# One block for both programs, a moved load, masks before scans, a later first scoring and eight more unit products in a fused linear-attention and two-MLP kernel

## The reference

```python
for t in range(S):
    state = alpha[:, :, t, :, None] * state + np.einsum('bhd,bhe->bhde', k[:, :, t], v[:, :, t])
    y[:, :, t] = np.einsum('bhd,bhde->bhe', q[:, :, t], state)
x = attn_out.transpose(0, 2, 1, 3).reshape(B * S, H * D)
h = x @ w_in;  g = h * np.clip(h + 3.0, 0.0, 6.0) / 6.0;  x = g @ w_out      # first MLP
h = x @ w_in2; r = np.maximum(h, 0.0); g = r * r;         out = g @ w_out2   # second MLP
```

## Time and profile before

| what | us |
|---|---|
| median of three timed executions | 908.76 |
| lowest, highest | 907.75, 910.27 |
| the profiled execution | 911.25 |
| its span, first to last instruction | 909.5 |
| TensorE busy (PE) | 892.4 |
| VectorE, ScalarE, GpSimd busy | 331.5, 337.1, 312.1 |
| mean granted clock of TensorE | 0.994 of full speed |

### The profile page before, as it was taken

How to read it: one execution, slowest core, us unless ns; L and a number is a source line. 1 busy time by engine, 2 the same in 40 slices (tenths; PEclk the granted TensorE clock), 3 DMA queues, 4 the chain that set the end, 5 groups by cost and what they waited for, 6 DMA issues and landing times.

```text
span 909.5 us, 12748 instructions
## 1 busy us (share of the span) xinstructions
PE 892.4 (98%) x5036; PEld 738.7 (81%) x5036; DVE 331.5 (36%) x498; ACT 337.1 (37%) x600; POOL 312.1 (34%) x246
## 2 busy tenths in 40 slices
PE   7889999999999999999999999999999999999997
PEld 7778888888888888788888888888888888888886
DVE  7667454534634543554233331221221221211211
ACT  3544433424334333333344543332333422423332
POOL 2534244324334342533233333233332323333232
PEclk9899999999999999999999999999999999999999
DMA  9922204212222232030022300000000000000000
GB/s 300 308 55 72 70 21 106 58 54 54 56 56 52 54 108 56 18 90 5 5 100 74 105 0 1 35 1 1 35 1 1 35 1 0 36 1 1 35 1 36
DMA packets 22363, 47.70 MB, mean 52 GB/s; under 512 B 3616, under 2 KB 10016, under 8 KB 22304
## 3 DMA queue, kind: packets, MB, share of 16 engines
q1 hardware_dynamic: 22304, 46.89, 17.4%
HBM read 40.19 MB, written 4.72 MB: 49 GB/s over the span
## 4 chain that ended last, share of the span: by engine, by line
PE 95%; DMA 2%; DVE 1%; issue 1%; ACT 1%; SPq 0%; DVEq 0%; ACTq 0%
PE h_ps L745 43%; PE o_ps L758 43%; PE att_ps L700 2%; PE att_ps L665 2%; PE att_ps L703 2%; DMA x_mid<-att_in 2%; PE att_ps L676 1%; PE att_ps L719 1%; DVE w_in_lo L579 0%; PE att_ps L686 0%; PE o_ps L665 0%; PE o_ps L686 0%; ACT w_in_hi L443 0%; DVE h_act L561 0%; DVE masked_t L534 0%
## 5 line engine op out<-in xcount | busy, mean ns | idle before, releaser
L360 POOL TENSOR_TENSOR g_parts<-h_act,g_parts 128x512 fp32r<-128x512 f32 x192 | 252.6, 1316 | 572.1 <-ACT g_parts L426 572.1
L758 PE MATMUL o_ps<-g_parts,w_out_hi 128*128 128x512 f32 x1152 | 327.0, 389 | 0.0
L745 PE MATMUL h_ps<-x_parts,w_in_hi 128*128 128x512 f32 x1152 | 297.5, 393 | 0.2 <-ACT x_parts L401 0.2
L758 PEld LDWEIGHTS o_ps<-g_parts,w_out_hi 128*128 128x128 f32 x1152 | 216.2, 188 | 45.0
L745 PEld LDWEIGHTS h_ps<-x_parts,w_in_hi 128*128 128x128 f32 x1152 | 213.0, 188 | 45.0 <-issue 0.7
L426 ACT ACTIVATE g_parts<-h_act 128x512 fp32r<-128x512 f32 x192 | 121.3, 632 | 292.6 <-PE o_ps L758 252.6
L564 DVE SCALAR_TENSOR_TENSOR h_act<-h_ps,h_gate 128x512 f32<-128x512 f32 x96 | 66.3, 691 | 290.5 <-ACT h_gate L421 290.5
L758 PE MATMUL o_ps<-g_parts,w_out_lo 128*128 128x512 f32 x576 | 165.6, 389 | 0.0
L745 PE MATMUL h_ps<-x_parts,w_in_lo 128*128 128x512 f32 x576 | 161.8, 389 | 0.0
L561 DVE SCALAR_TENSOR_TENSOR h_act<-h_gate,h_ps 128x512 f32<-128x512 f32 x96 | 65.7, 685 | 184.6 <-ACT h_gate L418 184.5
L745 PEld LDWEIGHTS h_ps<-x_parts,w_in_lo 128*128 128x128 f32 x576 | 108.1, 188 | 22.7
(11 more groups left out here) (89 smaller groups left out, 415.8 us busy)
## 6 DMA issues: line engine op xcount, KB each, us to landing
inputs<-att_in SPq DMA_DIRECT2D x20, 451.5 KB, 4.3
inputs<-att_in SPq DMA_DIRECT2D x20, 448.0 KB, 5.6
w_in_raw<-w_in SPq DMA_DIRECT2D x8, 768.0 KB, 8.4
w_out_raw<-w_out SPq DMA_DIRECT2D x8, 768.0 KB, 10.8
result<-inputs SPq DMA_DIRECT2D x18, 256.0 KB, 2.3
inputs<-v_in SPq DMA_DIRECT2D x20, 192.0 KB, 5.6
x_parts<-tails SPq DMA_DIRECT2D x120, 16.0 KB, 2.8
x_mid<-att_in SPq DMA_DIRECT2D x4, 451.5 KB, 7.5
```

Of the source, the lines that this page charges most:

```text
L360: nc.gpsimd.tensor_tensor(g_parts[:, g % 2, 1, :], h_act[:, g % 2, :], g_parts[:, g % 2, 0, :].bitcast(F32), ALU.subtract).then_inc(g_lo, 1)
L745: last = nc.tensor.matmul(h_ps[g % 2][:, :], w[:, m, cols], x_parts[:, n % 2, part, m, :], start=m == 0 and i == 0, stop=m == KT - 1 and i ...
L758: return nc.tensor.matmul(o_ps[m][:, :], w[:, f, m * P:(m + 1) * P], g_parts[:, g % 2, part, :], start=f == 0 and w is w_out_hi and part = ...
```

## The change

Five edits are made together.

1. Both programs are put in one block. `recurrent_program` no longer has its own; each engine waits for the judged flag, loads it and jumps, directly behind its own last work of the tiled program. SyncE waits for the stores at the very end. If the flag is set, the engines count themselves in (`all_engines`) before they start the second program.
2. On SyncE the loads of tile 3's decays and keys are issued ahead of the first group of weights.
3. In VectorE's step `make_decays` comes behind `decay_state`, `mask`, `x_low` and `update_state`.
4. Tiles 4 to 7, those scored during the first block, are scored at steps 3, 6, 9 and 12 instead of 2, 5, 8 and 11, and all that is tied to the scoring moves with it.
5. A fourth entry of `WARM_UP` puts eight unit products between tile 2's `turn_keys` and tile 3's `score`.

```diff
+FIRST_SCORE_AT = (3, 6, 9, 12)
-WARM_UP = (16, 8, 5)
+WARM_UP = (16, 8, 5, 8)
@@ build_program
-        chunked_program(nc, att_in, v_first, v_in, w_in1, w_out1, w_in2, w_out2, out, out_of_range)
-        recurrent_program(nc, raw, out, out_of_range)
+        out_stored = outer.enter_context(nc.semaphore("out_stored"))
+        range_judged = outer.enter_context(nc.semaphore("range_judged"))
+        semaphores = outer.enter_context(ExitStack())
+        block = outer.enter_context(nc.Block())
+        chunked_program(nc, block, semaphores, ...)
+        recurrent_program(nc, block, semaphores, raw, out, out_of_range, out_stored, range_judged)
@@ tiles_at
-            scored_in = [(n * FT + SCORE_AT[c], BATCH * (n + 1) + c) for n in range(NBLK - 1) for c in range(BATCH)]
-            return [t for at, t in scored_in if max(at + after, 0) == g]
+            scored_in = [(n * FT + (SCORE_AT if n else FIRST_SCORE_AT)[c], BATCH * (n + 1) + c)
+                         for n in range(NBLK - 1) for c in range(BATCH)]
+            return [t for at, t in scored_in if at + after == g]
@@ SyncE
-            load_w(0)
             load_decays(3)
             load_keys(3)
+            load_w(0)
...
-            sp.wait_ge(out_stored, 16 * KT * NBLK)
@@ VectorE, step g
-                for t in tiles_at(g, -DECAYS_LEAD):
-                    make_decays(t)
                 for t in tiles_at(g, 0):
                     decay_state(t)
                     mask(t)
@@
                     if t < TILES - BATCH:
                         update_state(t)
+                for t in tiles_at(g, -DECAYS_LEAD):
+                    make_decays(t)
@@ TensorE
             turn_keys(2)
+            warm_up(3)
             score(3)
@@ recurrent_program
-        block = ctx.enter_context(nc.Block())
+        chunks_done = sem("chunks_done")
+        def out_of_range_on(engine):
+            engine.wait_ge(range_judged, 3)
+            return engine.value_load(out_of_range[0:1, 0:1], min_val=0, max_val=1) > 0
+        def all_engines(engine):
+            engine.sem_inc(chunks_done, 1)
+            engine.wait_ge(chunks_done, 5)
@@ each engine of it, here SyncE
-            with sp.If(sp.value_load(out_of_range[0:1, 0:1], min_val=0, max_val=1) > 0):
+            with sp.If(out_of_range_on(sp)):
+                sp.wait_ge(out_stored, ALL_STORED)
+                all_engines(sp)
...
+            sp.wait_ge(out_stored, ALL_STORED)
```

More of the change, by code:

```diff
@@ L38 @@
 IN_W = ATT_W + DM
+ALL_STORED = 16 * KT * NBLK
 PAD_W = 2 * KT * P
@@ L84, in build_program, with chunked_program @@
         out_of_range = outer.enter_context(nc.sbuf_tensor("out_of_range", [1, 1], mybir.dt.int32))
-        chunked_program(nc, att_in, v_first, v_in, w_in1, w_out1, w_in2, w_out2, out, out_of_range)
-        recurrent_program(nc, raw, out, out_of_range)
-def chunked_program(nc, att_in, v_first, v_in, w_in1, w_out1, w_in2, w_out2, out, out_of_range):
+        out_stored = outer.enter_context(nc.semaphore("out_stored"))
+        range_judged = outer.enter_context(nc.semaphore("range_judged"))
+        semaphores = outer.enter_context(ExitStack())
+        block = outer.enter_context(nc.Block())
+        chunked_program(nc, block, semaphores, att_in, v_first, v_in, w_in1, w_out1, w_in2, w_out2, out, out_of_range,
+                        out_stored, range_judged)
+        recurrent_program(nc, block, semaphores, raw, out, out_of_range, out_stored, range_judged)
+def chunked_program(nc, block, semaphores, att_in, v_first, v_in, w_in1, w_out1, w_in2, w_out2, out, out_of_range,
+                    out_stored, range_judged):
     with ExitStack() as ctx:
@@ L104, in sem @@
         def sem(name):
-            return ctx.enter_context(nc.semaphore(name))
+            return semaphores.enter_context(nc.semaphore(name))
         w_in_hi = sb("w_in_hi", [P, KT, FF], F32R)
@@ L232, in chunked_program @@
         x2_lo = sem("x2_lo")
-        out_stored = sem("out_stored")
         TAIL_MOVES = 2 * KT
@@ L817, in _, with recurrent_program @@
                     nc.tensor.matmul(att_ps[0][0:1, 0:1], in_range_all[:, :], ones[:, :], start=True, stop=True).then_inc(range_counted, 1)
-def recurrent_program(nc, raw, out, out_of_range):
+def recurrent_program(nc, block, semaphores, raw, out, out_of_range, out_stored, range_judged):
     q, k, v, alpha, w_in1, w_out1, w_in2, w_out2 = raw
@@ L895, in _ @@
                 sp.wait_ge(tile_stored, 16 * (2 * TILES + 1))
+            sp.wait_ge(out_stored, ALL_STORED)
         @block.gpsimd
         def _(pool):
-            with pool.If(pool.value_load(out_of_range[0:1, 0:1], min_val=0, max_val=1) > 0):
+            with pool.If(out_of_range_on(pool)):
+                all_engines(pool)
                 nc.gpsimd.memset(eye[:], 0.0).then_inc(eye_made, 1)
@@ L906, in _ @@
         def _(dve):
-            with dve.If(dve.value_load(out_of_range[0:1, 0:1], min_val=0, max_val=1) > 0):
+            with dve.If(out_of_range_on(dve)):
+                all_engines(dve)
                 nc.vector.memset(col_ones[:, :], 1.0).then_inc(vec_step, 1)
@@ L936, in _ @@
         def _(act):
-            with act.If(act.value_load(out_of_range[0:1, 0:1], min_val=0, max_val=1) > 0):
+            with act.If(out_of_range_on(act)):
+                all_engines(act)
                 with act.Fori(0, SEQ) as t:
@@ L975, in _ @@
         def _(pe):
-            with pe.If(pe.value_load(out_of_range[0:1, 0:1], min_val=0, max_val=1) > 0):
+            with pe.If(out_of_range_on(pe)):
+                all_engines(pe)
                 with pe.Fori(0, SEQ) as t:
```

1 line of the change is left out of this document (removed).

## The result

The changed kernel took 900.96 us, median of four executions (900.89 to 901.02), against 909.33 us for the kernel before in the same job (907.75 to 910.27): a ratio of 0.991, 95% interval 0.9893 to 0.9927. It was forecast as faster, at 898.8 us with a range of 895.5 to 903.5. The direction and the range held. The measured time is 2.2 us above the point forecast: of the 10.0 us expected between the medians 8.4 came; the two profiled executions (911.25 and 900.95 us, spans 909.5 and 899.2) are 10.3 apart.

The account below looks back on a forecast made before the run. TensorE, busy 98% of the span, was taken to bind. Terms 3.4 + 4.8 + 1.5 + 1.5 = 11.2 us took the profiled 911.25 to 900.05; the middle between that and 897.6 gave 898.8, range 895.5 to 903.5.

Parts of the forecast that it names:

- start of the loop (load, products): Ahead of the loop: its first product starts at 29.25 instead of 32.67, 3.4 us gained, bounds 0.3 and 4.1.
- loop: tile 4's wait and clock, later tiles: TensorE's waits for masks: 4.8 us at tile 4 (3.2 wait, 1.6 clock) and 1.5 us at later tiles.
- Load ahead: Tile 3's decays land earlier, but GpSimd holds VectorE's scan, which ends near 20.15 instead of 20.81: 0.65 us.
- Unit products: Ahead of tile 3's scores: they fill TensorE's 2.10 us wait and keep the clock high, delaying the scores 0.4 us.
- Masks and step: Loop step 3: scans leave the place before the masks, the later step adds room; 4.8 us, bounds 0 and 5.8.
- One block: Program's end: flag reads hide behind the last stores and one meeting of engines remains; 1.5 us, bounds 0.7 and 1.6.
- The median: Whole kernel: 900.05 us, or 897.6 if the median's 2.5 us offset is the profiler's own cost; the middle, 898.8, taken.
- The clock did not fall in the first stage: Rival: ahead of the loop the clock falls anyway, 3.1 of the 3.4 us are missing, 901.9 us; chance 13%.
- the wait at tile 4 did not move: Rival: the wait at loop step 3 moves instead of going, 1.5 to 3 us, 900.3 to 903.4 us; chance 10%.
- TensorE waits for no activation: Rival: scans behind masks make activations late at 15 tiles, costing 15 us, 913.8 us; chance 3%.
- that the one block changes nothing: Rival: at the program's end each engine's flag load shows somewhere, 1.5 us less gain, 900.3 us; chance 5%.

Follow-up runs that it names:

- u_warm: The changed kernel without the eight unit products ahead of tile 3's scores: 899.87 us.
- n_scale: The changed kernel with GpSimd scaling tile 4 in step 0 of the loop, as before the change, its scores still at step 3: 900.89 us.
- u_step: The changed kernel with the first block scored at steps 2, 5, 8 and 11 again, masks still ahead of the scans: 901.01 us.
- t_pe: The changed kernel, but TensorE waits for all stores before it reads the flag and jumps: 901.29 us.
- n_warm4: The changed kernel with four unit products instead of eight ahead of tile 3's scores: 900.85 us.
- n_best: The changed kernel without the eight unit products and with GpSimd scaling tile 4 in step 0: median 901.04 us.

## Why the prediction was right, point by point

The profiled spans differ by 10.3 us where 11.2 was the sum:

| term | said | between the profiles |
|---|---|---|
| start of the loop (load, products) | 3.4 | 3.40 (32.67 to 29.27) |
| loop: tile 4's wait and clock, later tiles | 4.8 + 1.5 | 6.46 (871.34 to 864.88) |
| end | 1.5 | 0.36 (5.40 to 5.04) |

*Load ahead.* Right in mechanism and size: the scan was held by GpSimd and ended at 20.16. Without the products the scores start at 23.42 (`u_warm`), 0.63 us before the 24.05 of the kernel before, where 0.65 was said. The trace agrees with the exclusive lock that the Trainium skill states (SBUF — State Buffer, on the shared port pair), and it does so again in `n_scale`, where the split is held for 2.2 us.

*Unit products.* The step "What they buy is the clock" gave them too much. The start came as said, but the move of the load alone gave it too (`u_warm`, 29.14). Their price was not the 0.4 us of delay named (it was 0.28 at the scores, 23.70 for 23.42, and 0.13 at the loop); it was 0.87 us at the other end of the program. And the 3.4 us of the start are counted against an execution in which the clock fell. With both edits undone it fell in the profiled execution, but two of four executions were as short as those of `u_warm`: there was no 3.4 us to gain in each execution.

*Masks and step.* The claim that the wait "ends even without the later step" is shown by `u_step`. The gain is the order's, 6.3 us with the clock (907.35 less 901.01), where 4.8 + 1.5 was said, and the step adds nothing to it.

*One block.* This is the term that was mis-sized: 0.36 instead of 1.5. The bounds, 0.7 to 1.6, did not hold it. The sum took the stores' issue and landing from the kernel before and let only the load of the flag vary. The fetch behind TensorE's jump came, and it was SyncE's store issue beside it that paid: 1.29 us instead of 0.43. Without a fetch the end goes from 5.40 to 4.17, which is 1.2 of the 1.5. The Trainium skill's rule (Runtime: NRT & Kernel Launch, on instruction fetch) names the engine that jumps as the one that stalls. The trace agrees that the jump brings a fetch, but shows hardly a stall of TensorE: its jump takes 0.36 us with the fetch and 0.23 without, and in `t_pe` the fetch starts only after TensorE's last instruction.

*The median.* The sum stood at 900.05 against the profiled execution, and the forecast went halfway to the median's offset, 1.25 us down. That was wrong: the profiled execution of the changed kernel, 900.95 us, is as long as its median. The offset went with the clock: 40 timed executions of the kernel before, in four jobs, run from 906.33 us with a mean clock of 0.999 to 912.00 with 0.993. The 900.05 with the end's 1.1 us less gain gives 901.2, and 900.96 was measured. So the point forecast missed by 2.2 us for two reasons that pull the same way, this step and the end. The result lies inside the range, but at the upper end of the 896.3 to 901 given as this case's own.

*Rivals.* The clock did not fall in the first stage, the wait at tile 4 did not move, and TensorE waits for no activation in the profile. The rival that got 5%, that the one block changes nothing, came nearest: 1.1 of its 1.5 us were missing, though not because a load of the flag showed.

## What to carry to other kernels

When two edits aim at one wait, undo each alone and both together: here the order of two calls on VectorE was all of it and the step none, and of load and unit products either held the clock in the profile. A wait of TensorE costs more than its length where the clock falls behind it, as it did here behind waits of 2.10, 2.55 and 3.12 us, so read the granted clock behind each such wait, and take a spread between the executions of one job (2.5 us before, 0.13 after) as a hint of it. At the end of a program every transfer counts, that of instructions too: a jump put beside the last stores can slow their issue, and here 32 instructions fewer ahead of the jump were enough to be rid of its fetch.

## What the runs showed of the hardware that was not expected

- A 16 KB fetch of instructions behind TensorE's jump lengthened an issue of a store on SyncE beside it: 1289 ns in the changed kernel, 1714 in `n_warm4`, 1042 in `n_scale` (there the third store), and 1042 to 1714 in all seven profiled kernels where it falls beside the stores. With the fetch elsewhere or absent no such issue takes over 433.
- The fetch starts 1.1 us after the jump (1.4 in `n_scale`), and TensorE hardly waits for it: its jump takes 365 ns with a fetch in the changed kernel and 227 without one in `u_warm`.
- 32 instructions fewer on TensorE ended that fetch, 0.87 us in all; 16 fewer did not.
- Two executions of `n_best` lost over a microsecond at a mean clock of 0.997 and 0.998, though TensorE's wait ahead of tile 3's scores was 1.4 us in the profiled one, as in `u_warm`, whose four executions stayed at 0.999 or above. What decides between them is open; those executions were timed without a profile, so where the clock fell is not known.
